# A fused attention, feed-forward and mixer kernel: splits and loads in another order, w_ch2 and h operands in other places, and the sums of h blocks on GpSimd

## The reference, cut to what matters

```python
def _moe2_ref(x, w_tok1, w_tok2, w_ch1, w_ch2):   # x: (4, 576, 512)
    xt = x.transpose(0, 2, 1)
    h = np.maximum(xt @ w_tok1, 0.0) @ w_tok2      # 576 -> 256 -> 576
    u = x + h.transpose(0, 2, 1)
    h2 = np.maximum(u @ w_ch1, 0.0) @ w_ch2        # 512 -> 1536 -> 512
    return u + h2
```

## Time and profile before

| | |
|---|---|
| Median of 3 runs | 744.74 us (740.33 to 745.08) |
| The profiled execution | 743.76 us |
| Its span, first to last instruction | 741.9 us |
| Mean granted TensorE clock | 0.954 |
| TensorE busy | 672.7 us (91%) |
| VectorE, ScalarE, GpSimd busy | 493.7, 320.2, 260.3 us |

### The profile page before, as it was taken

How to read it: one execution, slowest core, us unless ns; L and a number is a source line. 1 busy time by engine, 2 the same in 40 slices (tenths; PEclk the granted TensorE clock), 3 DMA queues, 4 the chain that set the end, 5 groups by cost and what they waited for, 6 DMA issues and landing times.

```text
span 741.9 us, 17173 instructions
## 1 busy us (share of the span) xinstructions
PE 672.7 (91%) x6977; PEld 647.4 (87%) x6977; DVE 493.7 (67%) x836; ACT 320.2 (43%) x676; POOL 260.3 (35%) x289
## 2 busy tenths in 40 slices
PE   8999999999999999994898788999697639999997
PEld 7879999999999999993787788999697639989997
DVE  5588876766777676782476767767386336574855
ACT  4573645354444534541442255636264224142530
POOL 5575746464646464611863411120301300000000
PEclk9999999999999999998899979999898959999999
DMA  9962433324323316229671343546786494969783
GB/s 192 252 140 51 79 66 55 63 54 88 61 55 62 75 38 127 79 63 177 144 262 65 125 164 123 189 145 217 237 266 228 151 373 166 232 258 243 240 236 65
DMA packets 210174, 109.46 MB, mean 148 GB/s; under 512 B 163112, under 2 KB 199088, under 8 KB 209584
## 3 DMA queue, kind: packets, MB, share of 16 engines
q1 hardware_dynamic: 200144, 103.06, 50.1%
q10 hardware_dynamic: 9952, 5.31, 3.0%
HBM read 69.41 MB, written 38.93 MB: 146 GB/s over the span
## 4 chain that ended last, share of the span: by engine, by line
PE 68%; DMA 10%; DVE 9%; SPq 6%; ACT 2%; POOL 2%; issue 2%; POOLq 0%; DVEq 0%
PE bank L961 8%; PE bank L963 7%; PE bank L962 7%; PE tq L961 3%; DMA ck__raw<-h_rows 3%; SPq L1835 3%; PE tq L962 3%; PE tq L963 3%; PE bank L837 2%; DMA W__raw<-in_moe_w_ch 2%; PE bank L1556 2%; PE bank L1016 2%; PE bank L1558 2%; PE bank L1557 2%; PE s L625 2%; PE tq L1556 2%
## 5 line engine op out<-in xcount | busy, mean ns | idle before, releaser
L1744 ACT ACTIVATE ck__hi<-ck__raw 128x576 fp32r<-128x576 f32 x84 | 51.4, 674 | 85.3 <-DMA ck__raw<-h_rows 85.3
L1748 DVE TENSOR_TENSOR ck__lo<-ck__raw,ck__hi 128x576 fp32r<-128x576 f32 x84 | 58.9, 747 | 37.8 <-ACT ck__hi L1744 37.8
L1556 PE MATMUL bank<-U__hi,W__hi 128*128 128x288 f32 x192 | 59.8, 312 | 17.9 <-ACT hq L1592 11.9
L1056 POOL TENSOR_TENSOR k_lo<-kr,k_hi 128x288 fp32r<-128x288 f32 x64 | 56.2, 882 | 25.4 <-ACT k_hi L1052 25.4
L1098 DVE RECIPROCAL rg<-rg 128x288 f32<-128x288 f32 x32 | 61.4, 1922 | 0.0
L1557 PE MATMUL bank<-U__hi,W__lo 128*128 128x288 f32 x192 | 58.8, 306 | 0.0
L1558 PE MATMUL bank<-U__lo,W__hi 128*128 128x288 f32 x192 | 58.5, 305 | 0.0
L961 PE MATMUL bank<-k_hi,WV_hi 128*128 128x288 f32 x184 | 55.5, 301 | 0.0
L1556 PEld LDWEIGHTS bank<-U__hi,W__hi 128*128 128x128 f32 x192 | 38.1, 199 | 19.1 <-ACT hq L1592 12.4
L962 PE MATMUL bank<-k_hi,WV_lo 128*128 128x288 f32 x184 | 54.3, 295 | 0.0
L963 PE MATMUL bank<-k_lo,WV_hi 128*128 128x288 f32 x184 | 54.1, 294 | 0.0
(11 more groups left out here) (253 smaller groups left out, 2341.2 us busy)
## 6 DMA issues: line engine op xcount, KB each, us to landing
h_rows<-hq SPq DMA_DIRECT2D x24, 1008.0 KB, 4.6
ck__raw<-h_rows SPq DMA_DIRECT2D x28, 864.0 KB, 5.5
W__raw<-in_moe_w_ch SPq DMA_DIRECT2D x7, 768.0 KB, 7.9
x_turned<-xblocks SPq DMA_DIRECT2D x16, 288.0 KB, 5.2
u_kept<-X SPq DMA_DIRECT2D x4, 1152.0 KB, 8.8
ub<-u_kept SPq DMA_DIRECT2D x4, 1152.0 KB, 6.9
xT_raw<-x_turned SPq DMA_DIRECT2D x4, 1024.0 KB, 5.8
out_x<-ob SPq DMA_DIRECT2D x56, 72.0 KB, 3.4
```

The source lines that it names most:

```text
L1056: e.tensor_tensor(lo, t, hi.bitcast(F32), ALU.subtract).then_inc(Z.lo_done, 1)
L1556: e.matmul(ps, wh[:, w], xh[:, x], start=not onto and kt == 0, stop=False, skip_group_check=onto)
L1744: e.activation(hi, raw, ACT.Copy).then_inc(Z.ch_done, 1)
L1748: e.tensor_tensor(lo, raw, hi.bitcast(F32), ALU.subtract).then_inc(Z.cl_done, 1)
```

## The change

1. **Token stage.** `xblocks3` gives batch 3 its own block buffer. `x_rows` is cut into `x_out` (store) and `x_in` (load), and the stores of batches 2 and 3 both stand ahead of the load of batch 2. The blocks of batch 1 stand three units earlier. Sums and splits of w_ch1 and u stand elsewhere: the sums of slab 0 are ahead of the splits of batch 1's rows, and each `x_parts(b)` is now between the two halves of `token_up(b-1)`.
2. **Sums.** The four h sums of a step go from VectorE to GpSimd. The u sums of batches 2 and 3, the sums of w_ch1's slab 2 and two of the w_ch2 sums go from GpSimd to VectorE.
3. **Waits.** A half product of a first step waits for the operand it uses, in place of one wait for all seven.
4. **w_ch2.** Other addresses (`W2_AT`, `CK_AT`). A11 and S1 with its partner are loaded behind steps 7 and 11, S4 and A22 only when the up stage is over; the splits of S3, S4 and A22 move into the down stage.
5. **h.** The buffers ck2 and ck3 lie in w_ch1's slab 1 and are loaded behind step 22, ahead of the last two h stores.

```diff
-        CK = [weights(f"ck{i}_", [P, NJ * HALF], (U0, U1)[i // 2] + 8 * NJ * HALF * (i % 2))[0] for i in range(NCK)]
+        W2_AT = [0, 8 * NJ * 2 * P, 16 * NJ * 2 * P, R0, R0 + 8 * NJ * 2 * P, U1, U1 + 8 * NJ * 2 * P]
+        CK_AT = [U0, U0 + 8 * NJ * HALF, R0 + NSL1, R0 + NSL1 + 8 * NJ * HALF]
...
-            return dict(gpsimd=gpsimd)
+            return dict(vector=queue) if s == NSL - 1 else dict(gpsimd=queue)
...
-        U_ORDER = (B11, T1_, B21, B22, T3_, T2_, T4_)
+            return dict(gpsimd=queue) if b < 2 else dict(vector=queue)
+
+        U_ORDER = (B11, T1_, T2_, B21, B22, T3_, T4_)
...
+                if j_ == 0:
+                    e.wait_ge(Z.ul_done, 7 * b_ + U_ORDER.index(i) + 1)
+                if b_ == 0 and j_ % 2 == 0:
+                    e.wait_ge(Z.w1_lo, 7 * (j_ // 2) + i + 1)
...
-                    if j == 0:
-                        e.wait_ge(Z.ul_done, 7 * (b + 1))
-                    if b == 0 and j % 2 == 0:
-                        e.wait_ge(Z.w1_lo, 7 * (j // 2 + 1))
...
-            def vector(e):
+            def gpsimd(e):
                 if q:
                     b11, b12, b22, b21, t1, t2, t4 = [h_slot(q - 1, i) for i in range(7)]
...
+                else:
+                    e.wait_ge(Z.p4_done, NQ)
+                    e.dma_start(tiles(W2[S4][2][:, :], NJ), w2_block(0, 1)).then_inc(Z.w2_in3, 16)
+                    e.dma_start(tiles(W2[A22][2][:, :], NJ), w2_block(1, 1)).then_inc(Z.w2_in3, 16)
...
+            return dict(vector=vector) if i in (S1, S2) else dict(gpsimd=gpsimd)
...
                 elif n < NCK:
-                    e.wait_ge(Z.p4_done, NQ)
+                    e.wait_ge(Z.p4_done, NQ - 2)
...
-                ff[d // 2 - 6].append(x_blocks(1, d))
-            ff[-31].append(x_rows(0))
-            ff[-4].append(x_rows(1))
+                ff[d // 2 - 9].append(x_blocks(1, d))
+            ff[-31] += [x_out(0), x_in(0)]
+            ff[-7].append(x_out(1))
+            ff[-1].append(x_in(1))
...
-            extra[15] += [load_w2(0)]
-            extra[16] += [w2_sums(0)]
+            extra[7].append(load_w2(0))
+            extra[11].append(load_w2(1))
+            extra[17].append(w2_sum(S1))
+            extra[18] += [w2_sum(S2), load_h(0), load_h(1)]
             for i in range(3):
-                extra[17 + i].append(w2_parts(i))
-            extra[18] += [load_h(0), load_h(1)]
-            extra[20] += [load_w2(1), w2_sums(1)] + [chunk_parts(g) for g in range(3)]
-            extra[21] += [w2_parts(3), chunk_parts(3)]
-            extra[22] += [load_w2(2), w2_sums(2), w2_parts(4), chunk_parts(4), chunk_parts(5)]
-            extra[23] += [w2_parts(5)]
-            extra[24] += [load_u(0), load_h(2), load_h(3), load_u(1)]
+                extra[19 + i].append(w2_parts(i))
+            extra[20].append(load_w2(2))
+            extra[22] += [load_h(2), load_h(3), w2_sum(S3)] + [chunk_parts(g) for g in range(3)]
+            extra[23] += [chunk_parts(g) for g in range(3, 6)]
+            extra[24] += [load_u(0), load_w2(3), load_u(1), w2_sum(S4), w2_parts(A12)]
```

More of the change, by code:

```diff
@@ L1318, in sync, with x_in @@
                     e.dma_start(rows_of[g], blocks).then_inc(xd_out[b], 16)
+            return dict(sync=sync)
+        def x_in(b):
+            raw = xTs[b][2]
+            def sync(e):
                 e.wait_ge(xd_out[b], 64)
@@ L1460, in load_w1, with w1_sum, queue @@
             return dict(sync=sync)
-        def w1_sums(s):
+        def w1_sum(s, k):
             raw = [w[2][:, :] for w in W1[s]]
[L1466 to L1472, removed]
-                e.tensor_tensor(raw[S4], raw[A12], raw[S2], ALU.subtract).then_inc(Z.w1_sums, 1)
-            return dict(gpsimd=gpsimd)
+            made, first = (Z.w1_last_sums, 0) if s == NSL - 1 else (Z.w1_sums, 4 * s)
+            def queue(e):
+                if k == 0:
+                    e.wait_ge(w1_in[s], 64)
+                    e.tensor_tensor(raw[S1], raw[S3], raw[A22], ALU.add).then_inc(made, 1)
+                elif k == 1:
+                    e.wait_ge(made, first + 1)
+                    e.tensor_tensor(raw[S2], raw[S1], raw[A11], ALU.subtract).then_inc(made, 1)
+                elif k == 2:
+                    e.wait_ge(made, first + 1)
+                    e.tensor_tensor(raw[S3], raw[A11], raw[S3], ALU.subtract).then_inc(made, 1)
+                else:
+                    e.wait_ge(made, first + 2)
+                    e.tensor_tensor(raw[S4], raw[A12], raw[S2], ALU.subtract).then_inc(made, 1)
+            return dict(vector=queue) if s == NSL - 1 else dict(gpsimd=queue)
         def w1_parts(s, i):
@@ L1658, in load_w2 @@
[L1658 to L1674 removed]
+                    e.wait_ge(Z.ul_done, 7 * 2)
@@ new lines, in load_w2, with w2_sum, vector, gpsimd @@
+            return dict(sync=sync)
+        def w2_sum(i):
+            raw = [w[2][:, :] for w in W2]
+            def vector(e):
+                if i == S1:
+                    e.wait_ge(Z.w2_in1, 32)
+                    e.tensor_tensor(raw[S1], raw[S1], a22_first[:, :], ALU.add).then_inc(Z.w2_sums, 1)
+                else:
+                    e.wait_ge(Z.w2_in0, 16)
+                    e.wait_ge(Z.w2_sums, 1)
+                    e.wait_ge(Z.ul_done, 7 * B)
+                    e.tensor_tensor(raw[S2], raw[S1], raw[A11], ALU.subtract).then_inc(Z.w2_sums, 1)
+            def gpsimd(e):
+                if i == S3:
+                    e.wait_ge(Z.w2_in2, 48)
+                    e.tensor_tensor(raw[S3], a11_again[:, :], raw[S3], ALU.subtract).then_inc(Z.w2_last_sums, 1)
+                else:
+                    e.wait_ge(Z.w2_in3, 32)
@@ L1935, in down_stage @@
             for g in range(chunks):
-                if g == 1:
-                    steps.append(w2_parts(6))
+                if g in (3, 9, 13):
+                    steps.append(w2_parts({3: S3, 9: S4, 13: A22}[g]))
                 while made < min(chunks, g + LEAD + 1):
```

159 lines of the change are left out of this document (75 added, 84 removed).

## The result

The changed kernel takes 704.64 us (median of 4 runs, 700.31 to 709.4), the kernel before 744.9 (4 runs, 740.33 to 745.08): a ratio of 0.9475 with a 95% interval of 0.9396 to 0.9554. The forecast was 694.7 with a range of 684 to 709. The profiled execution is one of the longer ones: 707.15 us, span 705.3.

What follows compares the result with a forecast made beforehand. The prediction took the loss to be queue order, not throughput, with TensorE waiting. 741.9 - 5 - 31.9 - 13.2 + 0 = 691.8 us, plus 1.9 and 1.0 from profiled span to median, gave 694.7 us, range 684 to 709.

Steps and rivals of the forecast that it cites:

- about 701: Upper one of the forecast's own ends for the whole kernel, in us; the lower was 684.
- S4 late: Rival, down stage: S4's load lands 3 us later, chunks 14 and 15 wait some 6 us; 703 us, chance 0.08.
- a token stage without gain: Rival: the token stage's new order gives nothing and the load for `ub` is slow; 705 us, chance 0.07.
- Token stage, -5: Token stage: the new order, with batch 1's rows there earlier, saves 5 us, bounds -1 and -9.
- the load lands no earlier than now: Token stage: batch 2's load, behind batch 3's store on SyncE, gains nothing; batch 2 loses 1 to 2 us.
- Up stage, -31.9: Up stage: 135.2 us without stalls plus 1.5 for slab 2, in place of 168.6; bounds -33.4 and -21.
- on the path they are at nothing: Up stage: h sums on GpSimd cost the path nothing as long as the slot they fill is stored in time.
- The cover of 2 us: Up stage: an h store lands at 10.0 us, its slot is written again at 12.0 us, so 2 us spare.
- the lock rival: Rival, up stage: GpSimd and VectorE block each other, stores come late, ScalarE and TensorE wait 18 us; 713 us, chance 0.12.
- To chunk 6, -13.2: From the up stage's end to chunk 6: 13.7 us where it was 26.95; bounds -17 and -9.
- Chunk 6 to the end, 0: Last stage, 135.75 us before: clock gives back 1 us, S4 costs 1, up to 5; net 0.
- Ahead of the token stage, 0: The 335.6 us before the token stage are left alone except for three transposes' places; no change.

Runs made afterwards that it cites:

- the two repeats: The changed kernel run again unaltered, twice: 703.75 us (ratio 0.9437) and 704.16 us (ratio 0.9473) against the kernel before.

## Why the prediction held, and where its terms were off

The measured 704.64 us lies in the range, but not by the forecast's own strength. It is 9.9 us over the forecast and above "about 701", which the forecast called its own upper end; the range reached 709 because it took in two rivals, S4 late and a token stage without gain, and neither came as described. Nor does the sum give 701: its own upper bounds make 741.9 - 1 - 21 - 9 + 5 + 2.9 = 718.8.

**Token stage, -5: measured -5.2** (75.0 to 69.8), and undoing this part alone gives 5.5 us back. The details were less good, so the match of the total is in part luck. The store did go out 4 us earlier, counted from the start of the stage, and batch 1's rows were to be there 8.7 us into it; their splits began at 350.45 - 339.6 = 10.8 us, where before it was 348.38 - 335.6 = 12.8. The stop for the second relu copy, behind those splits, was taken at 2.7 us and was 6.36. By batches TensorE's gaps shrank by 2.6 us (10.07 to 6.36 and 1.10), where 3 to 4 had been forecast, shrank by 2.0 (2.88 to 0.87 in two), where 3 had been, and grew by 0.5 (2.83 to 3.33 in two), where 1 to 2 had been; the errors offset each other. In the two repeats the gap left in the second batch was 2.43 and 1.39 us. TensorE's time without work still fell from 75.0 - 58.1 = 16.9 us to 69.8 - 57.8 = 12.0. And "the load lands no earlier than now" for batch 2 was read as harmless. It held the stage once the splits were out of the way (5.84 us), and it was avoidable: the store of batch 3 had no need to go first.

**Up stage, -31.9: measured -28.3.** The steps are 5.6 us as computed (adds of VectorE start at 506.28 and 511.88), slab 2's late sums cost 0.5 us at 421.14 where I had taken 1.5, and the stalls for w_ch2 are gone. The slot waits, 3.8 us on TensorE, are about the 3.6 us that are missing. The step that failed is "on the path they are at nothing" for the h sums. The cover of 2 us was worked out from the median store of 4.6 us; near the loads of w_ch2 and ck a store took up to 8.8. That was the lock rival's consequence by another cause: the sums are 0.80 us as assumed in the steady steps, and the cover is eaten by DMA traffic. GpSimd's longer time for the four sums comes on top: with VectorE's sums the same traffic (4.2 to 9.9 us for a store) costs TensorE 1.1 us and not 3.8. With the h sums on VectorE the stage is 1.9 to 3.3 us shorter. (The 1.2 us that the prediction gives VectorE ahead of GpSimd's start are 2.05 - 0.46 = 1.6 by its own rows; nothing hangs on it.)

**To chunk 6, -13.2: measured -11.3.** The chain was the forecast one, sum of S3, eight h sums, store, `ub`. Counted from the end of the up stage, the last sum ended 6.8 us behind it and not 4.7: 0.80 us for each h sum was right alone, 1.2 to 2.2 beside VectorE's splits. The load took 7.6 us, within what was assumed. The chain was also avoidable: `ub` waited for the last store by its place in SyncE's queue alone.

**Chunk 6 to the end, 0: measured +4.2, in the two repeats +2.6 and +3.7.** I had expected S4's delay at chunks 14 and 15. It came at chunk 12 (1.96 us), where two ck4 splits that start late run beside S4's second sum and take 3.23 us. Another 2.0 us is the same 936 matmuls being busy for 129.97 us in place of 128.00, at a granted clock of 0.96 against 0.98, and 0.3 us are two older gaps. The clock was expected to give back 1. Behind the gap at chunk 6, now shorter, it did recover sooner (a granted clock of 0.77 in the first 6 us, 0.52 before); but it fell to its lower level again behind the gap at chunk 12, and behind one of 1.89 us at 615.63, where before, behind 1.74 us at 653.87, it had stayed high:

```profile
615.63:652.24 36.61, 35.33 (x252) 35.12 (x253) 22.77 (x40) 12.85 (x22) 0.00 (x0) 0.95 0.76 231
```

```profile
653.87:688.84 34.97, 33.81 (x253) 33.60 (x253) 22.60 (x40) 12.81 (x22) 0.00 (x0) 1.00 0.79 240
```

The first row is of the changed kernel, the second of the kernel before, in the columns of the earlier trace rows. Why the one gap brought the clock down and the other did not, no run shows.

**Ahead of the token stage, 0: measured +4.0** in the first trace, -1.1 in the second and +0.3 in the third. That is the scatter of the early clock.

The forecast of the profiled span was 691.8; the three traces have 705.3, 698.7 and 702.6. Their errors add up as 3.6 (up), 1.9 (chunk 6), 4.2 (the end) and 4.0 (scatter) for the first, less 0.2: 13.5. Three terms were off in the same direction. The first two, and the gap at chunk 12, are prices that had been read alone and that neighbours raised: DMA traffic for the stores, VectorE's splits for the h sums, S4's sum for the ck splits. The rest of the last term is the clock.

**The rule.** The trace shows two ck splits or three going on for the length of the GpSimd sum beside them (5.92 for 2.09 us), and a GpSimd h sum of 0.80 us at 2.21 behind VectorE's splits. That is what the Trainium skill states (SBUF — State Buffer, section "SBUF: two separate sides"): the pair is a lock, and the loser waits in full. I had weighed it at a chance of 0.12 because the steady steps leave room for both engines, and there they do. The places where it costs are those with large sums of w_ch2. The second rule of the Trainium skill (GPSIMD Engine Reference, section "Engine selection"), that elementwise work belongs on VectorE, as GpSimd is about twice as slow with two inputs, agrees with the trace: 0.46 us against 0.80 for the same sum. The kernel with the h sums on VectorE has the lower median by 4.3 us, with intervals that overlap, and the shorter up stage.

**What the change did.** None of its gain comes from moving the h sums. The kernel with every other part and the h sums where they were is at 0.9377, the h sums alone are at 1.0287, and together they make 0.9437. Of the other parts only the token stage's order was undone by itself, for 7.7 of some 41 us. The rest was not separated: the w_ch2 loads' new places and addresses, the waits per operand, the earlier loads of ck2 and ck3, and the sums that went to VectorE. That the w_ch2 stalls of 536.95 and 566.04 went with the order of its loads is read from the traces, and not shown by a run that moves those alone.

## What to carry to other kernels

Before work is moved to an engine with free time, ask whether the full one was late: VectorE was busy for 118 of 168.6 us in the kernel before, and with about the same work, 113 us, in another order, the stage took 138.6. A cover computed from a median transfer is gone in the steps where loads are in flight; take the longest one there. Where a gap closes and the time stays, look for the next input in the trace of the new kernel, not the old one: here the rows of one batch hid behind splits, and one transfer's place in SyncE's order took 7.0 us off the stage where moving the splits had left it within 1 us.

## What was not expected of the hardware

- GpSimd loses to VectorE as well: an h sum of 0.80 us alone took 1.2 to 2.2 us beside VectorE's splits, while a long sum of 3.4 to 3.5 us took 3.47 to 3.90 and held up VectorE's splits for about its own length.
- VectorE's adds that read PSUM took 0.44 to 0.46 us each in the three stages, beside GpSimd or not.
- Four transfers of the turned blocks (288 KB each) took 5.3 to 9.6 us to issue, and eight took 15.5 to 17.5, while the three transfers of a load of the rows took 1.7 to 2.9: what stands behind such stores in SyncE's queue waits for their issue.
- TensorE's granted clock from 20 to 36 us was 0.68, 1.00 and 1.00 in three traces of one kernel, and the token stage of the first began 3.7 to 5.1 us later.
